# Bank X of the fourth-quarter sum read by VectorE out of PSUM, in place of a ScalarE copy and a GpSimd sum

## What is computed

```python
h = (x @ w1) * (x @ w2)              # gates, 512 -> 1024
x = (h @ w3) @ w_out                 # computed as h @ (w3 @ w_out)
p = domain_probs / (domain_probs.sum(-1, keepdims=True) + 1e-9)
for e in range(4):                   # experts
    out += p[:, e:e+1] * (np.maximum(x @ w1[e], 0) @ w2[e])
```

## Time and profile before

| | us |
|---|---|
| median of 3 runs | 987.01 (986.8 to 987.72) |
| the profiled execution | 987.27, of which the span is 985.5 |
| TensorE busy | 976.9 (99%) |
| VectorE busy | 621.5 (63%) |
| ScalarE busy | 453.0 (46%) |
| GpSimd busy | 403.8 (41%) |
| granted TensorE clock | 1.0 in all slices |

### The profile page before, as it was taken

The page is one execution under the profiler, slowest core; times in us unless marked ns, Lnnn a source line. Parts: engine busy times, 40 slices in busy tenths (PEclk is TensorE's granted clock), DMA queues, the critical chain, the costliest instruction groups (busy, mean ns, idle before and its releaser), DMA issues.

```text
span 985.5 us, 15682 instructions
## 1 busy us (share of the span) xinstructions
PE 976.9 (99%) x5398; PEld 906.6 (92%) x5398; DVE 621.5 (63%) x948; ACT 453.0 (46%) x837; POOL 403.8 (41%) x380
## 2 busy tenths in 40 slices
PE   9999999999999999999999999999999999999998
PEld 6889999999989999999998988989989899898997
DVE  5359999999987994798754362543534535254442
ACT  4248888888875443554541330413304234042230
POOL 1103433437697990885162250522604216043130
PEclk9999999999999999999999999999999999999999
DMA  7335555655432220101110201002010011100102
GB/s 247 113 88 129 143 130 131 149 123 133 121 97 75 68 80 1 44 23 43 44 41 3 65 23 43 27 17 64 23 43 21 21 54 31 39 26 21 43 24 104
DMA packets 81965, 66.87 MB, mean 68 GB/s; under 512 B 32896, under 2 KB 67840, under 8 KB 81920
## 3 DMA queue, kind: packets, MB, share of 16 engines
q1 hardware_dynamic: 81920, 66.29, 24.6%
HBM read 44.20 MB, written 3.19 MB: 48 GB/s over the span
## 4 chain that ended last, share of the span: by engine, by line
PE 64%; POOL 1%; issue 0%; ACT 0%; DVE 0%; POOLq 0%; ACTq 0%
PE ps L295 21%; PE ps L296 21%; PE ps L297 21%; POOL w_raw L586 0%; POOL c L654 0%; POOL w_raw L590 0%; POOL a L639 0%; ACT w_hi L744 0%; POOL c L639 0%; POOL v_sum L633 0%; ACT kept L822 0%; POOL w_raw L593 0%; DVE acc L1293 0%; POOLq L492 0%; POOL w_raw L587 0%
## 5 line engine op out<-in xcount | busy, mean ns | idle before, releaser
L633 POOL TENSOR_TENSOR v_sum<-kept,kept 128x384 f32<-128x384 f32 x48 | 51.9, 1081 | 286.7 <-ACT kept L822 286.7
L822 ACT COPY kept<-ps 128x384 f32<-128x384 f32 x144 | 67.6, 478 | 203.1 <-PE ps L297 202.1
L1293 DVE SCALAR_TENSOR_TENSOR acc<-ps,gate,acc 128x512 f32<-128x512 f32 x96 | 72.0, 750 | 139.7 <-PE ps L297 139.7
L297 PE MATMUL ps<-v_hi,hid_lo 128*128 128x512 f32 x384 | 149.6, 390 | 0.0
L296 PE MATMUL ps<-v_lo,hid_hi 128*128 128x512 f32 x384 | 149.5, 389 | 0.0
L295 PE MATMUL ps<-v_hi,hid_hi 128*128 128x512 f32 x384 | 149.4, 389 | 0.0
L1006 DVE TENSOR_SCALAR_CACHE_REDUCE expo<-ps 128x768 f32<-128x768 f32 x96 | 91.7, 956 | 14.2 <-PE ps L1404 10.6
L719 ACT ACTIVATE expo<-expo,neg_max 128x768 f32<-128x768 f32 x96 | 90.5, 943 | 7.8 <-DVE expo L1006 5.7
L1020 DVE TENSOR_TENSOR pT_lo<-ps,pT_hi 128x768 fp32r<-128x768 f32 x96 | 90.5, 947 | 4.9 <-ACT pT_hi L733 4.2
L1142 DVE TENSOR_TENSOR u_sum<-ps,kept 128x384 f32<-128x384 f32 x48 | 26.6, 554 | 100.5 <-PE ps L297 100.5
L733 ACT CAST pT_hi<-ps 128x768 fp32r<-128x768 f32 x96 | 76.6, 798 | 26.4 <-PE ps L1415 26.0
(11 more groups left out here) (158 smaller groups left out, 2512.7 us busy)
## 6 DMA issues: line engine op xcount, KB each, us to landing
w_raw<-in_moe_w SPq DMA_DIRECT2D x64, 128.0 KB, 2.4
e_raw<-in_moe_w SPq DMA_DIRECT2D x64, 128.0 KB, 2.4
v_raw<-in_moe_w SPq DMA_DIRECT2D x32, 256.0 KB, 3.5
w_raw<-in_moe_w SPq DMA_DIRECT2D x8, 512.0 KB, 3.9
raw_qk<-in_q SPq DMA_DIRECT2D x16, 192.0 KB, 3.1
raw_qk<-in_k SPq DMA_DIRECT2D x16, 192.0 KB, 3.4
raw_v<-in_v SPq DMA_DIRECT2D x16, 192.0 KB, 3.2
k_main<-q_main SPq DMA_DIRECT2D x16, 192.0 KB, 2.5
```

The costliest lines, as they stand in the source:

```text
L297: return nc.tensor.matmul(out_ps, lhs_lo, rhs_hi, start=False, stop=stop, skip_group_check=onto)
L633: nc.gpsimd.tensor_tensor(v_sum[:, :], kept[s][1][:, :], kept[s][2][:, :], ALU.add).then_inc(v_done, 1)
L822: nc.scalar.copy(kept[s][n][:, :], ps[4 * s + n][:, 0:HALF]).then_inc(kept_done, 1)
L1293: nc.vector.scalar_tensor_tensor(acc[:, t, :], ps[4 * ((h + t // 4) % 2) + t % 4], gate_f[:, bass.ds(t * E + e, 1)], acc[:, t, :], ALU.mul ...
```

## The change

ScalarE copies only banks A and Y (`kept` has two buffers a set, and `kept_done` counts two a step). `sum_kept` goes from GpSimd. VectorE makes `v_sum` itself, bank X read out of PSUM plus `kept` of Y, right before `sum_u`; it waits for the third product, for the copy of Y and for `c22_done`. TensorE's S4 onto bank X waits for `v_done` in place of the third copy. On GpSimd the even gate step's last quarter waits for `ab22_done` of the pair before, since `a22` is read by it.

```diff
-        kept = [[place(f"kept{n}_{s}", [P, HALF], F32) for n in range(3)] for s in range(2)]
+        kept = [[place(f"kept{n}_{s}", [P, HALF], F32) for n in range(2)] for s in range(2)]
@@ GpSimd
-            def sum_kept(step, s):
-                pool.wait_ge(kept_done, 3 * step + 3)
-                if not isinstance(step, int) or step:
-                    pool.wait_ge(c22_done, step)
-                held()
-                nc.gpsimd.tensor_tensor(v_sum[:, :], kept[s][1][:, :], kept[s][2][:, :], ALU.add).then_inc(v_done, 1)
...
                     a, unit = GATE_STEPS * b + 2 * i, FG * b + i
-                    sum_kept(a, 0)
-                    if not unit:
+                    if unit:
+                        pool.wait_ge(ab22_done, unit)
+                    else:
                         pool.wait_ge(x_scaled, 2 * PAIRS)
                     last_quarter(a, a22)
                     combine_gate(a + RAWS)
-                    sum_kept(a + 1, 1)
...
-                        sum_kept(step, (h + j) % 2)
@@ ScalarE
             def keep(step, s, pieces=(), r=0):
-                for n in range(3):
+                for n in range(2):
@@ VectorE
+            def sum_v(step, s):
+                dve.wait_ge(prod, N_PROD * step + 3)
+                dve.wait_ge(kept_done, 2 * step + 2)
+                if not isinstance(step, int) or step:
+                    dve.wait_ge(c22_done, step)
+                nc.vector.tensor_tensor(v_sum[:, :], ps[4 * s + BANK_X][:, 0:HALF], kept[s][1][:, :], ALU.add)\
+                    .then_inc(v_done, 1)
+
             def sum_u(step, s):
                 dve.wait_ge(prod, N_PROD * step + 4)
-                dve.wait_ge(kept_done, 3 * step + 1)
+                dve.wait_ge(kept_done, 2 * step + 1)
                 if not isinstance(step, int) or step:
-                    dve.wait_ge(c22_done, step)
                     dve.wait_ge(c12_done, step)
...
+                    sum_v(a, 0)
                     sum_u(a, 0)
...
+                sum_v(a + 1, 1)
                 sum_u(a + 1, 1)
...
+                        sum_v(step, s)
                         sum_u(step, s)
@@ TensorE
-                    if second:
-                        pe.wait_ge(kept_done, 3 * step + bank + 1)
+                    if second and bank == BANK_X:
+                        pe.wait_ge(v_done, step + 1)
+                    elif second:
+                        pe.wait_ge(kept_done, 2 * step + bank + 1)
```

## The result

| | before | after |
|---|---|---|
| median, us | 987.01 (11 runs, 985.84 to 989.63) | 988.98 (11 runs, 988.72 to 990.18) |
| profiled execution's span, us | 985.5 | 987.1 |
| gates of batch 0, lost by TensorE | 1.08 | 3.25 |
| gates of batch 1, lost | 0 | 1.01 |
| step 16 to the last matmul (experts) | 497.2 | 497.2 |

The ratio is 1.0022 [1.0014, 1.0029]: 2 us slower, just outside the 0.2% that a measurement tells from no change, though the interval reaches inside it. "Lost" is the time from the first matmul of step 1 (of step 8 in batch 1) to `multiply_y`'s first, less the stage's undisturbed length (51.74 us for steps 1 to 7, 59.14 for steps 8 to 15, which the kernels that lose nothing show).

The account below looks back on a forecast made before the run. TensorE was taken as the bound, with VectorE and GpSimd full beside it in the gates. Batch 0's +1.9 and batch 1's +0.5 sum to +2.4 us, 989.7 against the profiled execution, so a median of 989.4; range 986.6 to 991.8.

Parts of the forecast that it names:

- case 1: Gates: VectorE late for bank X, so S4 waits; 988.2 to 991 us, likeliest 989.4; chance 0.63.
- The new wait: S4 waits for VectorE's `v_sum` in the gates: +1.9 us in batch 0, +0.5 in batch 1.
- The relief: Gates: with GpSimd's `v_sum` gone, VectorE gets back 0.44 us a step, against 0.47 added.
- rival 3: Gates: no relief for VectorE, GpSimd stays full; +7.0 us, 994.0; chance 0.12.
- The proportion: VectorE's loss in the gates falls by the 18% of GpSimd's work that the two `v_sum` are.
- Its 4.9 us: VectorE's loss per pair of gate steps from stretched `w_lo` and `hid_lo` beside GpSimd.
- rival 2: Gates: relief keeps pace, `v_sum` is in time and the 1.07 us stall goes; 986.0 to 987.7; chance 0.23.
- Batch 1: Gates, step 13: S4 late by +1.1 us plus +0.1 drift, taken at half, +0.5; bounds 0 and +2.5.
- The stall of before: Gates of batch 0: TensorE's wait at 355.70, fifth product of step 7, goes: up to -1.07 us.
- Experts at zero: 32 expert steps: `v_sum` fits into VectorE's idle time with 2.4 us to spare; zero.
- `multiply_y`, ScalarE, the dropped waits at zero: `multiply_y` covered by late need of `hid_lo`, ScalarE's 48 fewer copies, waits dropped on GpSimd: each zero.

Follow-up runs that it names:

- run 3: The changed kernel plus an unused GpSimd sum of two SBUF buffers in each gate step where the old sum stood; 993.05 us, ratio 1.0057.
- run 6: The changed kernel once more, unchanged, for a second profile; 988.95 us, ratio 1.0025.
- runs 4 and 10: 4: changed kernel, `v_sum` moved between the two `w_lo` parts, 985.45 us; 10: kernel before, first gate combines ahead of GpSimd's last scaling of x, 985.51 us.
- run 2: The changed kernel with VectorE's `v_sum` made from ScalarE's SBUF copies and S4 waiting for the third copy again; 986.84 us, ratio 0.9994.

## Why the prediction was right, and where not

The forecast was 989.4 and case 1; measured 988.98, by that mechanism.

- **The new wait.** Right: TensorE waits for `v_sum` before S4 in steps 3 to 7, most in odd ones, and the wait for `kept` is gone. The even steps' waits are smaller than the 0.3 us foretold, 0.12 and 0.13. S4 of step 7 was to come 51.76 + 1.67 + 0.2 = 53.63 us after step 1's start, and came at 53.83 (358.44 - 304.61). `multiply_y` was to start 54.7 us after step 1 and did at 55.0. `v_sum` itself started 53.23 us after step 1 (357.84 - 304.61) where 52.74 + 0.2 was taken, 0.3 us more drift; the release took 0.05 us, not the 0.14 borrowed from ScalarE's. Behind the wait came 0.10 for the slower product, which no term held.
- **The relief.** Taken as 0.44 us a step from GpSimd's 18%; the pair's period gives (0.94 + 0.05) / 2 = 0.50, the `w_lo` alone 0.52, and run 3, which takes the relief away, lands near rival 3's price. The proportion was a good guide. Its 4.9 us left out VectorE's two products of SBUF operands, which take 0.65 and 1.02 us in the stretch (L1179, L1186) and 0.56 alone; with them the loss is 5.5 us a pair and the proportion gives the measured 0.50. The Trainium skill (SBUF — State Buffer, section Who interferes with whom) speaks of an exclusive lock between GpSimd and VectorE's instructions with two SBUF inputs. The trace agrees: `w_lo` became shorter as GpSimd's work went, and `v_sum` and `u_sum`, with one input in PSUM, stay at 0.54 to 0.56 us throughout. A removed GpSimd sum of 1.02 us gave back half its length, though, not all of it, as rival 2 in its whole-length form would have had.
- **Batch 1, mis-sized.** The rows gave 1.1; I halved it to 0.5 for a relief "likelier above the proportion here". It lost 1.01, 0.96, 1.01 and 0.99 in four profiles of the new gates. That halving is the term that was mis-sized, by half: one stretched `v_sum` at 435.17 was given more weight than the sum worked out from starts.
- **The stall of before, mis-read, and luck in the total.** "The 1.07 us stall goes" is right, but 1.07 was one execution's, with GpSimd early. A second profile of the same kernel shows 3.32. The forecast of +2.4 to the first profile was borne out only against a profile of the changed kernel with GpSimd as early (run 6): 3.51 - 1.08 = +2.43, made of +1.47 in batch 0 and +0.96 in batch 1 where +1.9 and +0.5 were foretold, two errors that cancel. Between the two first profiles the gates differ by 3.18, and the executions by only 1.7, because step 1 came 1.52 us earlier. So the mechanism was right, and that the median came within 0.5 us is in part luck. Rival 2's line that "there is just 1.07 us to win" was too tight as well: the medians of runs 4 and 10 lie 1.5 below.
- **Experts at zero.** Right to 0.1 us. `v_sum` took idle time there and `u_sum` still waits for TensorE; VectorE's timeline, first step of a round:
```profile
551.88 0.56 DVE L1134 TENSOR_TENSOR v_sum<-ps,kept 128x384 f32<-128x384 f32 x1 [2.43 <-PE ps L298]
...
552.94 0.56 DVE L1143 TENSOR_TENSOR u_sum<-ps,kept 128x384 f32<-128x384 f32 x1 [0.50 <-PE ps L298]
```
- **`multiply_y`, ScalarE, the dropped waits at zero.** Right: `multiply_y` takes 33.3 us in both.

## What to carry to other kernels

An addition that reads a bank ties TensorE to the queue of the engine that makes it. Ask not only whether that engine has the time, but what stands in front of the instruction when TensorE needs the bank: the same 16 additions leave 3.5 us or more lost behind both parts of a `w_lo`, and nothing between the two parts. Work taken from an engine that is full but not the bound is worth what its neighbour gets back, here half of its length, and only as long as the neighbour's new work comes in time. And a stall of 1 us seen in one profile may be a phase: where an engine enters a full stretch just behind a DMA round trip, profile the kernel twice, and put work that doesn't need the DMA ahead of it.

## What the runs showed of the hardware

- The small store and reload of the reciprocals varied from one execution to the next: GpSimd stood idle for it for 6.70 us in one profile of the old kernel and 8.08 in another, from the same point before step 1 (11.64 us). It cost the first combine 1.05 us of its lead, and TensorE lost 2.2 us more.
- With its first loads from DRAM TensorE gets to its 78th matmul 17.9 to 19.9 us after the start, whatever the kernel (14 profiles). This moves the span by up to 2 us, as much as the change does; stages must be compared from their own starts.
- A product whose first matmul had waited takes 1.13 to 1.17 us where others take 1.056.
- From the end of VectorE's `v_sum` to the matmul that waited for it are 0.05 us (22 waits in six profiles), from ScalarE's `kept` 0.14 (12 waits). It isn't a matter of the engine: behind VectorE's `w_lo` (343.51, run 2) it is 0.15 too. Why is open.
